# Gate products of an attention-and-experts kernel, written as two products of 64 stationary columns

## The reference

```python
# 4 batches, 8 heads, 576 tokens, head size 64
scores = (q @ k^T) / 8 - slope[h] * |i - j|       # only 0 <= i - j < 128
attn   = softmax(scores);  x = attn @ v           # heads side by side: 2304 x 512
# first mixture: 8 experts, one per token
e = argmax(x @ w_gate);  x = max softmax * relu(x @ w1[e]) @ w2[e]
# second mixture: 4 experts, all of them, weighted by domain shares p
out = sum_e p[:, e] * relu(x @ w1'[e]) @ w2'[e]
```

## Time and profile before

| what | value |
|---|---|
| median of 3 runs | 1215.9 us |
| profiled execution | 1217.94 us |
| its span in the trace | 1216.3 us |
| PE busy | 1193.7 us (98%), 6446 matrix passes |
| DVE busy | 735.6 us (60%) |
| POOL busy | 796.0 us (65%) |
| ACT busy | 419.3 us (34%) |
| gate products | 80, of which 64 have 128 stationary columns; 160 passes |

### The profile page before, as it was taken

The page is one execution under the profiler, slowest core; times in us unless marked ns, Lnnn a source line. Parts: engine busy times, 40 slices in busy tenths (PEclk is TensorE's granted clock), DMA queues, the critical chain, the costliest instruction groups (busy, mean ns, idle before and its releaser), DMA issues.

```text
span 1216.3 us, 18893 instructions
## 1 busy us (share of the span) xinstructions
PE 1193.7 (98%) x6446; PEld 1051.8 (86%) x6447; DVE 735.6 (60%) x1604; ACT 419.3 (34%) x766; POOL 796.0 (65%) x523
## 2 busy tenths in 40 slices
PE   8999999999999999999999999999999999999997
PEld 7888887788888888989889999999999999999996
DVE  7888977222222247666666666666666666666664
ACT  5655651121211243333333333333333333333330
POOL 5465684856666765558758776678578676666652
PEclk9999999999999999999999999999999999999999
DMA  7855777878888703212221132121211221111101
GB/s 278 277 201 198 284 264 260 332 287 323 320 315 319 295 27 123 73 48 84 75 70 70 70 115 102 70 87 52 96 70 70 76 92 63 65 70 70 70 36 52
DMA packets 46636, 177.79 MB, mean 146 GB/s; under 512 B 9313, under 2 KB 15585, under 8 KB 30177
## 3 DMA queue, kind: packets, MB, share of 16 engines
q1 hardware_dynamic: 29680, 121.57, 27.9%
q0 software_dynamic: 7520, 43.07, 9.6%
q10 hardware_dynamic: 9360, 12.17, 3.0%
HBM read 157.51 MB, written 19.36 MB: 145 GB/s over the span
## 4 chain that ended last, share of the span: by engine, by line
PE 93%; DVE 3%; DMA 1%; POOL 1%; issue 1%; ACT 0%; POOLq 0%; ACTq 0%; SPq 0%; DVEq 0%
PE ps L1821 33%; PE ps L1764 29%; PE ps L1681 9%; PE ps L1665 9%; PE ps L1588 5%; PE ps L1571 2%; PE ps L1692 1%; PE ps L1559 1%; PE ps L1560 1%; PE ps L1602 1%; PE ps L1620 1%; DVE qk_split L1099 1%; DMA x_rows<-x_by_expert 1%; DMA qk_raw<-q_k_turned 1%; DVE scores_probs L1137 1%
## 5 line engine op out<-in xcount | busy, mean ns | idle before, releaser
L1514 DVE SCALAR_TENSOR_TENSOR out_sums<-ps,share_token,out_sums 128x512 f32<-128x512 f32 x270 | 202.5, 750 | 134.4 <-PE ps L1821 133.2
L1764 PE MATMUL ps<-x_hi,w_hi 128*128 128x384 f32 x672 | 225.6, 336 | 2.4 <-DVE sum_u L1476 2.4
L1821 PE MATMUL ps<-w_hi,h_hi 128*128 128x512 f32 x576 | 226.7, 394 | 0.0
L1821 PE MATMUL ps<-w_hi,h_lo 128*128 128x512 f32 x576 | 226.3, 393 | 0.0
L1821 PE MATMUL ps<-w_lo,h_hi 128*128 128x512 f32 x576 | 225.9, 392 | 0.0
L1764 PE MATMUL ps<-x_lo,w_hi 128*128 128x384 f32 x672 | 225.4, 335 | 0.0
L1764 PE MATMUL ps<-x_hi,w_lo 128*128 128x384 f32 x672 | 225.3, 335 | 0.0
L744 POOL TENSOR_TENSOR w_lo<-w_raw,w_hi 128x1024 fp32r<-128x1024 f32 x48 | 115.4, 2404 | 163.4 <-ACT w_hi L1005 163.4
L622 POOL TENSOR_TENSOR w_split<-w_raw,w_split 128x2048 fp32r<-128x2048 f32 x31 | 142.5, 4603 | 64.2 <-DMA w_split<-weights 41.8
L1032 ACT ACTIVATE h_hi<-ps 128x384 fp32r<-128x384 f32 x192 | 90.4, 493 | 210.1 <-DVE ps L1483 155.7
L739 POOL TENSOR_TENSOR w_lo<-w_raw,w_hi 128x1024 fp32r<-128x1024 f32 x48 | 116.0, 2417 | 55.1 <-ACT w_hi L1016 55.0
(11 more groups left out here) (229 smaller groups left out, 1921.9 us busy)
## 6 DMA issues: line engine op xcount, KB each, us to landing
w_raw<-weights SPq DMA_DIRECT2D x80, 1024.0 KB, 4.7
w_split<-weights POOLq DMA_DIRECT2D x32, 1024.0 KB, 7.6
qk_raw<-q_k_turned SPq DMA_DIRECT2D x16, 1152.0 KB, 6.3
v_one<-v_ones SPq DMA_DIRECT2D x16, 365.0 KB
y_sorted<-y ACTq DMA_DIRECT2D x20, 256.0 KB, 2.9
x_rows<-x_by_expert ACTq DMA_DIRECT2D x19, 256.0 KB, 4.4
v_t<-v_turned SPq DMA_DIRECT2D x16, 288.0 KB, 6.4
x_by_expert<-zeros SPq DMA_DIRECT2D x16, 260.0 KB, 7.5
```

What stands on the lines that cost most here:

```text
L1514: v.scalar_tensor_tensor(out=a_, in0=ps[:, 4 + t % 3, :], scalar=share_, in1=a_, op0=ALU.mult, op1=ALU.add).then_inc(acc_done, 1)
L1764: last = mm(ps[:, bank, 0:HALF_T], wt[:, w, c * P:(c + 1) * P], xt[:, c, x, :], start=(k == 0), stop=(k == 3 * KC - 1))
L1821: last = mm(ps[:, 4 + t % 3, :], ht[:, f, t * P:(t + 1) * P], wt[:, f, :], start=(k == 0), stop=(k == n - 1))
```

## The change

```diff
-                ins = mm(ps[0:ROWS[t], 6 + k, t * VG_N:(t + 1) * VG_N], vt_sb[:, k, t * P:t * P + ROWS[t]],
-                         wg_sb[:, n % PAIRS * 2 * E1:n % PAIRS * 2 * E1 + VG_N], start=True, stop=True)
+                for half in range(ROWS[t] // DH):
+                    ins = mm(ps[half * DH:(half + 1) * DH, 6 + k, t * VG_N:(t + 1) * VG_N],
+                             vt_sb[:, k, t * P + half * DH:t * P + (half + 1) * DH],
+                             wg_sb[:, n % PAIRS * 2 * E1:n % PAIRS * 2 * E1 + VG_N], start=True, stop=True)
```

## The result

The changed kernel takes 1227.05 us, the median of 6 runs (1226.23 to 1230.32). The kernel before, in 6 runs beside it and earlier, has 1216.03. The ratio is 1.0088, with a 95% interval of 1.0075 to 1.0101, so the change costs 9 to 12 us. The profiled execution takes 1227.09 us against 1217.94, which is 9.2 more. I had forecast +17.5. The sign was right, and the size was off by more than a third: the time stands at the very edge of my range.

A forecast was written before the change was run, and what follows sets the result against it. PE, busy for 98% of the span, was taken to bound the kernel. 21.3 us for 14 pairs + 0.2 at the start - 4.0 given back = +17.5 us, from 1215.9 to 1233.4 us; range 1227 to 1241 for 8 in 10.

The forecast's parts named there:

- points 1 and 2: All four split gate products, tiles 0 to 3, pay for entering and leaving the narrow form: 0.94 us a pair.
- point 3: Second half's two more passes on PE: 0.144 us, bounded by 0 and 0.25; 0.58 for four tiles.
- E: Not slower: the split halves run side by side, filling the array without a gap; 1212 us, or 1219; chance 0.05.
- D: DVE sets the attention's pace, hiding part of the cost: 1226 us; chance 0.08, including halves fully side by side.
- point 5: PE gets back two waits and a slow-clock stretch in the attention: 0.88 + 1.52 + 1.6 = 4.0 us.
- point 4: 14 pairs pay in full, 21.3 us; products of pairs 0 and 1 before 17 us let 0.2 us through.
- wait at 143.99: PE's wait for a split on POOL, 0.88 us, expected to go.
- slow clock: PE's half clock behind the second wait, lasting about 3.4 us and costing about 1.6, expected to go.
- wait for the ranks: PE's wait at 159.37 us for the copy of the ranks, a DVE operation: 1.52 us, expected to go.
- B: Halves of split gate products run one after another, 0.125 us a pass: +23.4, 1239.3 us; chance 0.21.
- C: PE's waits stay, the DVE operation meeting a POOL split again, clock falling behind: 1237 us; chance 0.18.

The follow-up runs named there:

- e4: Kernel before, with the fifth tile's gate product padded from 64 to 128 stationary columns with zeros; 1215.01 us, ratio 0.9970.
- e8: Changed kernel, with the upper halves moved behind the transposes of the same turn, lower halves left in place; 1245.15 us, ratio 1.0207.
- e2: Changed kernel, with the lower half's product issued twice in a row, then the upper one; 1233.74 us, ratio 1.0131.
- e11: Kernel before, with the last pair's tile 0 gate product issued one duo later, beside that of tile 1; 1218.59 us, ratio 0.9982.
- e12: Changed kernel, with the last pair's tile 0 gate product issued one duo later, beside that of tile 1; 1228.11 us, ratio 1.0061.
- e7: Changed kernel, with a pair's five gate products grouped in tile 0's duo, between narrow transposes and narrow products with v; 1215.36 us, ratio 0.9966.
- e5: Changed kernel, with a pair's five gate products grouped where the fifth tile's stood, for pairs 1 to 15; 1220.70 us, ratio 1.0006.
- e10: As e5 on the changed kernel, but pair 1's gate products stay spread over duos 1 to 4; 1218.43 us, ratio 0.9982.
- e9: As e7 on the changed kernel, but the last pair's group of gate products comes two duos later; 1215.35 us, ratio 0.9952.

## Why the prediction was wrong in size

**Which places pay, and the price of entering and leaving (points 1 and 2): right.** 0.94 us a pair was forecast from the tile-4 product, 0.98 was measured: tiles 0, 2 and 3 at 0.26, 0.26 and 0.24 as worked out, tile 1 at 0.21 instead of 0.18, the upper end of what its bounds gave. e4 takes the same price away from the one product that paid it before, and e8 pays it again where the upper half stands alone.

**The price of the second half (point 3): the step that failed.** I took 0.144 us from bounds of 0 and 0.25, and it is 0: 14 x 0.58 = 8.1 us of the forecast don't exist. My reading of the tile-4 product was sound, with one exposed load and then passes of 0.07 us, and e2 shows just that price. What I carried over wrongly was that the second half queues behind the first as a second product on the same columns would. It doesn't even wait for the first half's second pass. The value I should have leaned to was the one in E and in D's parenthesis. It is also what the Trainium skill ("TensorEngine Tiling (Array Packing)", Key Properties) says of tiles that run in parallel, and here the trace agrees, with pairs of loads and passes 0.006 us apart. With it the sum is 13.2 + 0.2 - 4.0 = +9.4 us, against 9.2 in the profiled execution. That this fits so closely is in part luck: 0.04 us a pair too little and 0.5 us too little in point 5 nearly cancel.

**How many are paid (point 4): 14 pairs by PE's own time, as counted.** The products ahead of them are nearly hidden as expected: the last scores of head 2 start at 15.0 us against 14.7.

**What PE gets back (point 5): 4.0 forecast, 4.5 measured** (14 x 0.98 less 9.2), but for a reason that I had only half. The wait at 143.99 (0.88 us) and the slow clock (about 1.6) went as forecast. Of the wait for the ranks 0.97 us went and 0.55 stayed: the DVE operation is slow again (3.42 us) and again ends with a POOL split. That the split is the cause wasn't tested. What I had left out makes up for it: a wait of 0.28 us for ACT at 177.76 is gone, and 0.9 us comes back behind the attention. And e11 shows that the wait for the ranks wasn't PE's to give back by itself, nor the slow clock with it.

**The rivals.** B, the halves one after another, is refuted by the four loads within 0.20 us. So is, for column groups, the rule of the Trainium skill ("TensorE: Matmul & The Clock Gate", Part 3, The mechanism) that loads overlap passes only where row groups differ: both halves use all rows, and the last load starts 0.06 us behind the first pass. C was right that the DVE operation meets a POOL split again, and wrong in its price: the wait is 0.55 us, and no slow clock follows. D was right about the place, the last pairs, and wrong about a third of the rest. E fell on the gap, which comes ahead of the split product as it does ahead of tile 4's, and was right that the halves run side by side.

**Left open.** How much of the difference between the ratio of all runs (+10.7 us) and the profiled pair (+9.2) is the stretch at half clock, which the profiled execution of the kernel before has and others may lack, wasn't settled. The times point that way. In the three later sets the runs of the kernel before with a mean clock of 0.997 or more have medians of 1216.1, 1217.2 and 1217.6 us, those with 0.995 or less 1218.1, 1220.2 and 1221.3. All six runs of the changed kernel have 0.997 or more. And e12, whose trace is within 0.3 us of the changed kernel's at the last scores, has a ratio of 1.0061 in its own set, +7.4 us. Open too is what TensorE does in the gaps, whether it waits until its array is empty or only holds the next load back; no run parts the two.

## What to carry to other kernels

In a stream of full-width float32 products, a product with 64 or 32 stationary columns costs 0.21 to 0.26 us more than the same product with 128, for entering and leaving the form, so padding a lone narrow product to 128 columns makes it faster (e4). Once in the narrow form, products on other column groups are free and the slot is shorter (0.074 us against 0.111), so narrow products pay in a group, best next to work that is narrow anyway (e7). Price a new pass by the columns that it shares with its neighbour, and before counting on a wait to go, look for the engine that is late next.

## What the runs showed of the hardware

- TensorE paired the halves though they stand one after another: written as lower and upper, each of two passes, they started as two pairs 0.006 us apart, loads included. In e2 an upper product was paired with a lower one across a repeated lower product between them (starts 0 and 0.014 us, the last alone at 0.274). For halves of one product this is inferred from the start times, since the trace doesn't name them. In groups of nine such products a pair of passes starts every 0.074 us, against 0.111 for full passes of the same 86 columns.
- Eight passes on four column groups took 0.35 us, no more than two passes on one (0.36).
- Float32r scores with 64 stationary columns make no gap on either side, while float32 products with 64 do, between float32r scores and between float32 products (e8). They aren't the only kind that pays: the transposes of a fifth tile have 64 contraction rows, and the first of them, with 128 stationary columns, starts 0.20 us behind the full transpose ahead of it, where full ones follow after 0.11. The last of them has 64 stationary columns too, and so adds to the narrow operations that are listed for the kernel before.
- The clock fell to half at 13.0 us in e5, where PE had been busy for 3.70 of the 6 us from 7 to 13, and not in e10, where it had been busy for 5.13. A stretch at half clock moved when a wait was taken away, and didn't vanish (e9, e11).
- A 64-column product ran beside an unrelated 64-column product on the other columns at no cost (e8, tile 0), and there the rows have names: gate, product with v, gate, product with v, at 46.32, 46.33, 46.45 and 46.47 us, though the code issues both gate passes first.
